# Score products in 64x64 tiles of the array, and the order of a step's work on TensorE, VectorE and ScalarE

## The reference

```
for t in range(S):
    kt, vt, rt = (k[:, :, t], v[:, :, t], r[:, :, t])
    cur = np.einsum('bhd,bhe->bhde', u[None] * kt, vt)
    y[:, :, t] = np.einsum('bhd,bhde->bhe', rt, state + cur)
    state = w[None, :, :, None] * state + np.einsum('bhd,bhe->bhde', kt, vt)
...
x = transposed y, (3072, 384)
logits = x @ phi; d = softmax over tokens; c = softmax over slots
slot_out[e] = relu(slot_input[e] @ w1[e]) @ w2[e];  x = c @ slot_out
h = x @ w_in;  g = h * (1.0 / (1.0 + np.exp(-1.702 * h)));  out = g @ w_out
```

## Time and profile before

| what | value |
|---|---|
| median of three runs | 389.57 us (388.96 to 389.83) |
| profiled execution | 389.61 us, its span 387.8 us, mean granted TensorE clock 0.996 |
| TensorE matmuls busy | 375.5 us, 97% of the span |
| VectorE, ScalarE, GpSimd busy | 229.2, 187.4, 111.7 us |
| moved by DMA | 63.77 MB, of which 58.75 MB read from HBM |
| attention | first 122 us; experts to about 160 us; feed-forward to the end |

### The profile page before, as it was taken

One profiled execution on the slowest core, in us unless ns is written; L12 is line 12 of the kernel. 1 busy time (PEld: TensorE's weight loads), 2 busy tenths in 40 slices (PEclk: granted clock), 3 DMA queues, 4 the chain that ended last, 5 costly groups with the idle time before them and its releaser, 6 DMA issues.

```text
span 387.8 us, 9112 instructions
## 1 busy us (share of the span) xinstructions
PE 375.5 (97%) x3224; PEld 296.0 (76%) x3224; DVE 229.2 (59%) x419; ACT 187.4 (48%) x432; POOL 111.7 (29%) x125
## 2 busy tenths in 40 slices
PE   7889899999999999899999999999999999999996
PEld 6778687877876344578888888888888888888885
DVE  6787778787774301286665565555556655655560
ACT  1235454545444431576655546454655465455552
POOL 5987798887682020144400000000000000000000
PEclk9899999999999999999999999999999999999999
DMA  7999999999999999900002001000200020002002
GB/s 232 289 315 394 382 355 405 403 370 358 402 336 370 328 334 403 378 26 3 0 0 84 0 0 67 16 0 0 81 0 0 0 81 0 0 0 81 0 2 82
DMA packets 28966, 63.77 MB, mean 164 GB/s; under 512 B 3088, under 2 KB 17056, under 8 KB 28560
## 3 DMA queue, kind: packets, MB, share of 16 engines
q1 hardware_dynamic: 27600, 62.99, 44.6%
q10 hardware_dynamic: 1344, 0.49, 0.7%
HBM read 58.75 MB, written 4.72 MB: 164 GB/s over the span
## 4 chain that ended last, share of the span: by engine, by line
PE 79%; DMA 7%; POOL 6%; issue 3%; DVE 2%; SPq 2%; ACT 0%; DVEq 0%; POOLq 0%
PE bank L598 11%; PE bank L597 11%; PE bank L596 11%; PE pair L596 6%; PE pair L598 5%; PE pair L597 5%; PE bank L341 5%; PE pair L380 4%; DMA ring<-win 4%; PE bank L583 4%; DMA krb<-kr 3%; PE pair L371 3%; PE pair L363 3%; PE bank L401 2%; POOL rkn L1046 2%
## 5 line engine op out<-in xcount | busy, mean ns | idle before, releaser
L825 DVE TENSOR_TENSOR gf<-bank,sg 128x512 f32<-128x512 f32 x72 | 49.7, 692 | 63.4 <-ACT sg L993 63.1
L993 ACT ACTIVATE sg<-bank 128x512 f32<-128x512 f32 x72 | 42.9, 598 | 73.3 <-PE bank L583 73.2
L597 PE MATMUL bank<-ghi,whi 128*128 128x512 f32 x192 | 74.7, 389 | 0.0
L596 PE MATMUL bank<-glo,whi 128*128 128x512 f32 x192 | 74.7, 389 | 0.0
L598 PE MATMUL bank<-ghi,wlo 128*128 128x512 f32 x192 | 74.7, 389 | 0.0
L831 DVE TENSOR_TENSOR glo<-gf,ghi 128x512 fp32r<-128x512 f32 x96 | 69.4, 723 | 0.2
L999 ACT ACTIVATE ghi<-gf 128x512 fp32r<-128x512 f32 x96 | 60.0, 625 | 0.9 <-DVE gf L825 0.8
L873 ACT ACTIVATE yt<-pair 112x512 f32<-112x512 f32 x24 | 14.3, 598 | 57.7 <-PE pair L380 57.7
L596 PEld LDWEIGHTS bank<-glo,whi 128*128 128x128 f32 x192 | 36.0, 188 | 7.5
L597 PEld LDWEIGHTS bank<-ghi,whi 128*128 128x128 f32 x192 | 36.0, 188 | 7.5
L598 PEld LDWEIGHTS bank<-ghi,wlo 128*128 128x128 f32 x192 | 36.0, 188 | 7.5
(11 more groups left out here) (162 smaller groups left out, 535.0 us busy)
## 6 DMA issues: line engine op xcount, KB each, us to landing
ring<-w SPq DMA_DIRECT2D x24, 512.0 KB, 6.3
rkb<-rk SPq DMA_DIRECT2D x23, 512.0 KB, 5.4
krb<-kr SPq DMA_DIRECT2D x24, 384.0 KB, 5.6
ring<-w SPq DMA_DIRECT2D x4, 1536.0 KB, 14.5
ring<-w SPq DMA_DIRECT2D x8, 768.0 KB, 10.4
vb<-v SPq DMA_DIRECT2D x24, 192.0 KB, 5.6
out<-ob SPq DMA_DIRECT2D x18, 256.0 KB, 2.1
ring<-win SPq DMA_DIRECT2D x3, 1024.0 KB, 14.1
```

The source lines that it names most:

```text
L596: pe.matmul(o, w_hi, lo, start=(f == 0), stop=False)
L597: pe.matmul(o, w_hi, hi, start=False, stop=False)
L825: dve.tensor_tensor(gf[:, f % 2, :], bank[f % 4][:, :], sg[:, f % 2, :], ALU.mult).then_inc(gf_ok, 1)
L993: act.activation(sg[:, f % 2, :], bank[f % 4][:, :], ACT.Sigmoid, scale=1.702).then_inc(sg_ok, 1)
```

## The change

The scores are cut into halves of their output partitions, 16 products of 48x64 instead of 8 of 48x128. The products of the earlier state with r (`earlier`) leave `outputs` and stand directly ahead of the scores of the next step. The transposes of the bonus values (`bonus_turns`) leave `outputs` too and come last in the step, behind tokens, for the step's own n. So the order becomes earlier(n-1), scores(n), values(n-1), state(n-1), tokens(n-2), bonus_turns(n), and at b = 2 the gathering behind that. Both new groups get waits of their own through an instruction that raises `tiles_go`. VectorE scales step n+1 ahead of the mask of n. ScalarE's decay comes ahead of its columns, and `row_exp` at the end of its step (5,3). GpSimd subtracts the row maximum ahead of the bonus values of (5,3); `vd` is released by a semaphore of its own, `vd_used`.

```diff
@@ scores
+                pe.sem_inc(tiles_go, 1)
                 for hp in range(HP):
-                    for p0, i in HEADS:
-                        s = slice(p0, p0 + D)
-                        last = pe.matmul(SC[i][:, hp * CH:(hp + 1) * CH],
-                                         rks[s, b % 2, 1, hp, :], rks[s, b % 2, 0, hp, :], start=True, stop=True)
+                    for half in HALVES:
+                        for p0, i in HEADS:
+                            s = slice(p0, p0 + D)
+                            last = pe.matmul(SC[i][half, hp * CH:(hp + 1) * CH],
+                                             rks[s, b % 2, 1, hp, half], rks[s, b % 2, 0, hp, :], start=True, stop=True)
...
+            def bonus_turns(c, b):
+                n = B * c + b
                 wait(pe, yt_ok, n)
                 wait(pe, vd_ok, n + 1)
...
+                last.then_inc(vd_used, 1)
+            def earlier(c, b):
+                if is_first(c):
+                    pe.sem_inc(rs_used, 1)
+                else:
+                    wait(pe, s_new, n - 2)
+                    pe.sem_inc(tiles_go, 1)
...
+                    last.then_inc(rs_used, 1)
...
@@ step on TensorE
+                if not is_first(c, b):
+                    earlier(*prev(c, b))
                 scores(c, b)
                 if not is_first(c, b):
+                    if is_first(c):
+                        bonus_turns(*prev(c, b))
                     outputs(*prev(c, b))
...
-                    if tail and b == 2:
-                        gather(c - 1, LG, 2 * c)
                     if not is_first(*prev(c, b)):
                         tokens(*prev(*prev(c, b)))
+                if not is_first(c) or b == B - 1:
+                    bonus_turns(c, b)
+                if tail and b == 2:
+                    gather(c - 1, LG, 2 * c)
...
@@ step on VectorE
+                if is_first(c) and b:
+                    mask(c, b)
+                    scale(*following(c, b))
+                else:
+                    if more:
+                        scale(*following(c, b))
+                    mask(c, b)
+                if more:
+                    bonus_sum(*following(c, b))
...
@@ step on ScalarE
-                if is_last(c) and b == 3:
-                    row_exp(0, EARLY)
                 if not is_first(c, b):
-                    columns(*prev(c, b))
                     if not is_last(prev(c, b)[0]):
                         decay(*prev(c, b))
+                    columns(*prev(c, b))
...
                         rows(*prev(*prev(c, b)))
+                if is_last(c) and b == 3:
+                    row_exp(0, EARLY)
...
@@ step on GpSimd
+                if is_last(c) and b == 3:
+                    pool.wait_ge(rmax_ok, 1)
+                    pool.tensor_tensor(*row_terms(0, 0, EARLY), ALU.subtract).then_inc(csub_ok, 1)
                 bonus_values(c, b)
```

More of the change, by code:

```diff
@@ L38 @@
 HEADS = ((0, 0), (64, 1))
+HALVES = (slice(0, 64), slice(64, P))
 LOWEST = -3.0e38
@@ L184, in rwkv_soft_moe_ffn @@
             sem(n) for n in ("zeroed", "chain", "tables", "wks_done", "wkn_ps", "wkn_ok"))
-        rks_ok, kk_ok, rk_ok, rku_ok, dd_ok, vd_ok, rs_used = (
-            sem(n) for n in ("rks_ok", "kk_ok", "rk_ok", "rku_ok", "dd_ok", "vd_ok", "rs_used"))
+        rks_ok, kk_ok, rk_ok, rku_ok, dd_ok, vd_ok, vd_used, rs_used = (
+            sem(n) for n in ("rks_ok", "kk_ok", "rk_ok", "rku_ok", "dd_ok", "vd_ok", "vd_used", "rs_used"))
         sc_ps, masked, yt_ps, yt_ok, st_ps, sdec, s_new, yn_ps, yn_ok = (
@@ L190, in rwkv_soft_moe_ffn @@
             sem(n) for n in ("lt_ps", "l_ok", "cm_ok", "nm_ok", "ex_ok", "al_ok", "tr_ps", "tr_ok", "p_ps", "run_ok"))
-        nm_new, l_new, mask_go = sem("nm_new"), sem("l_new"), sem("mask_go")
+        nm_new, l_new, mask_go, tiles_go = (sem(n) for n in ("nm_new", "l_new", "mask_go", "tiles_go"))
         spr_ok, bc_ps, nf_ok, fac_ok, lf_ok, ls_ps, samef_ok, rden_ok, si_ps, si_ok = (
@@ L229, in prev, with following @@
             return (c, b - 1) if b else (c - 1, B - 1)
+        def following(c, b):
+            return (c, b + 1) if b < B - 1 else (c + 1, 0)
         def is_first(c, b=0):
@@ L337, in scores @@
                 wait(pe, rks_ok, 2 * n + 2)
+                pe.sem_inc(tiles_go, 1)
                 for hp in range(HP):
-                    for p0, i in HEADS:
-                        s = slice(p0, p0 + D)
-                        last = pe.matmul(SC[i][:, hp * CH:(hp + 1) * CH],
-                                         rks[s, b % 2, 1, hp, :], rks[s, b % 2, 0, hp, :], start=True, stop=True)
-                        if hp == HP - 1:
-                            last.then_inc(sc_ps, 1)
+                    for half in HALVES:
[3 more added lines that the diff above has]
+                                             rks[s, b % 2, 1, hp, half], rks[s, b % 2, 0, hp, :], start=True, stop=True)
+                            if hp == HP - 1 and half == HALVES[1]:
+                                last.then_inc(sc_ps, 1)
                 if is_first(c, b):
@@ L350, in scores @@
                     keep_warm(LG, 4)
-            def outputs(c, b):
+            def bonus_turns(c, b):
                 n = B * c + b
-                if not is_first(c):
-                    wait(pe, s_new, n - 2)
                 wait(pe, yt_ok, n)
@@ L374, in outputs @@
                                                  start=False, stop=False, skip_group_check=True)
-                last.then_inc(rs_used, 1)
+                    last.then_inc(rs_used, 1)
+            def outputs(c, b):
+                n = B * c + b
                 wait(pe, masked, 2 * n + 2)
@@ L465, in spread_weights @@
                 last.then_inc(ct_ps, 1)
+            earlier(C - 1, B - 1)
             outputs(C - 1, B - 1)
@@ L737, in step @@
                 tail = not is_first(c)
[L738 to L750, removed]
+                more = not (is_last(c) and b == B - 1)
                 if tail and b == 1:
                     slot_max(c - 1)
+                if is_first(c) and b:
[7 more added lines that the diff above has]
+                    bonus_sum(*following(c, b))
                 if tail and b == 3:
                     running(c - 1)
-                if not is_first(c, b):
-                    if not is_first(*prev(c, b)) and not is_last(prev(*prev(c, b))[0]):
-                        new_state(*prev(*prev(c, b)))
+                if not is_first(c, b) and not is_last(prev(c, b)[0]):
+                    new_state(*prev(c, b))
                 if is_last(c) and b == 2:
@@ L761, in step @@
                     row_sum(*early)
+            scale(0, 0)
+            dve.tensor_tensor(wks[a, :, :], wk[a, :, :], pw[a, 7, :].unsqueeze(2).to_broadcast([PAIR, HP, CH]),
+                              ALU.mult).then_inc(wks_done, 1)
+            bonus_sum(0, 0)
             steps(dve, step)
-            mask(C - 1, B - 1)
             def low_weights(which, t):
@@ L1059, in bonus_values @@
                 pool.wait_ge(v_in[b], 16 * (c + 1))
-                wait(pool, rs_used, n - 1)
+                wait(pool, vd_used, n - 1)
                 if is_first(c, b):
@@ L1082, in step @@
                         pool.memset(own[:, j, 2, :].bitcast(F32), 0.0).then_inc(own_ok, 1)
-                if is_last(c) and b == 2:
-                    pool.wait_ge(rmax_ok, 1)
-                    pool.tensor_tensor(*row_terms(0, 0, EARLY), ALU.subtract).then_inc(csub_ok, 1)
                 if is_last(c) and b == 3:
```

## The result

The changed kernel takes 391.32 us (median of 8 runs, 389.36 to 392.67) where the kernel before takes 389.36 (8 runs, 388.71 to 389.85): a ratio of 1.0046, 95% interval 1.0027 to 1.0066. It is slower by 0.5%, where 0.9% faster was forecast.

The account below looks back on a forecast made before the run. TensorE was taken to set the pace in attention, DMA 6% behind. Gains of 3.3 + 0.8 + 0.15 - 0.65 = 3.6 us from 389.6 gave 386.0 us; own range 383.8 to 387.8, with rivals 382.6 to 389.2.

Parts of the forecast that it names:

- The step and the chunk: TensorE in attention: a step falls from 4.16 to 3.86 us, a chunk from 18.64 to 17.55 us.
- The rival of tiles two at a time: Scores of each step: half tiles run two at a time, 1.76 us instead of 0.88, kernel about 400 us; chance 0.06.
- The three changes of shape: TensorE's step: tile shape changes three times instead of five, 0.16 us each.
- (c) of the waits: ScalarE's step: decay ahead of columns ends at 1.7 us, columns can start at 2.6, so the order is free.
- The rival that DMA keeps the gain: Attention chunks: DMA holds 391 GB/s, not 403; chunk 18.1 us, kernel 388.2, or 389 with later `krb`; chance 0.22.
- The early part: Chunk from 31 to 51 us and all before it: 0.8 us won, bounds 0 and 2.
- The last chunk: Hidden transposes win 0.15 us; a new wait of about 1.4 us for GpSimd before the weights' transposes loses 0.65.
- The hand-over as a block: From SyncE's restart to `win` landing: 24 us of SyncE and DMA move with the time TensorE reaches the experts.
- The sum: Whole kernel: three chunks, early part, hidden transposes and end wait add to 3.6 us won, giving 386.0 us.
- `tiles_go`: Rival in each step: its two instructions hold back loads, costing what two shape changes saved; 390.2 us; chance 0.08.

Follow-up runs that it names:

- e4: Changed kernel with ScalarE's copy of the outputs (columns) ahead of the decay again in every step; 392.15 us, ratio 1.0041.
- e5: Changed kernel with both order edits, early softmax moved forward at the end and columns ahead of the decay, half scores kept; 391.73 us, ratio 1.0052.
- e9: e6 with 32 added instructions a step on TensorE's queue that only raise a semaphore nobody waits for; 453.48 us.
- e2: Kernel before with its scores alone as 16 products of 48x64, in the old place, with one semaphore instruction ahead; 390.77 us, ratio 1.0022.
- e11: e6 with the values' products cut in two along the tokens, 32 instructions more a step; 391.1 us, ratio 1.0045.
- e1: Changed kernel with its scores as 8 products of 48x128 again, all else as changed; 390.33 us, ratio 1.0005.
- e6: Changed kernel with early softmax moved forward at the end, columns ahead of the decay, and whole 48x128 scores; 388.51 us, ratio 0.9985.
- e12: e6 without the one semaphore instruction a step ahead of the scores; 388.69 us, ratio 0.9999.
- e10: e6 measured again, unchanged; 388.8 us, ratio 0.9990 to the kernel before.
- e8: Changed kernel with half tiles only in steps of even b, whole ones in odd b; 389.91 us, ratio 1.0019.
- e7: Changed kernel with the five pieces of `w1` of chunk 1 asked for behind the last step instead; 392.12 us, ratio 1.0050.
- e3: Changed kernel with the end's early softmax moved forward: ScalarE's exponential first in step (5,3), VectorE's row sum ahead of the running sums; 390.2 us, ratio 1.0024.

## Why the prediction was wrong, point by point

**The step and the chunk: right, one wait missed.** Start to start, earlier products and scores were to take 1.48 us:

```profile
81.67 0.66 PE L383 MATMUL pair<-rks,st 48*48 48x128 f32 x16
...
82.15 1.05 PE L347 MATMUL bank<-rks 48*64 48x128 f32 x32
...
83.13 1.08 PE L395 MATMUL pair<-at,vb 128*48 128x128 f32 x16
...
84.04 0.53 PE L407 MATMUL bank<-vb,kk 128*48 128x48 f32 x16
...
84.50 0.60 PE L416 MATMUL bank<-idt,yt 112*128 112x112 f32 x4
...
84.99 0.65 PE L366 MATMUL pair<-idt,vd 128*112 128x128 f32 x4
```

They take 1.46, and the 32 half tiles run four at a time, 0.98 us. The rival of tiles two at a time, 1.76 us, is out. The rule of the Trainium skill (TensorE: Matmul & The Clock Gate, Part 3, The mechanism), by which the two halves of a head would not overlap, does not agree with this trace. The three changes of shape came as counted.

The chunk was forecast at 17.55 and measured at 17.9, which takes some 1 us from the gain of the three. The missing 0.35 is in the b = 1 step, in (c) of the waits, where I called the decay ahead of the columns free. That holds where ScalarE is idle, not behind the logits:

```profile
55.19 1.00 POOL L1063 TENSOR_TENSOR rkn<-krb 128x384 f32<-128x384 f32 x1
55.23 0.97 DVE L744 TENSOR_TENSOR stat<-stat 128x1 f32<-128x1 f32 x1
...
56.24 0.37 ACT L919 ACTIVATE et<-bank,stat 128x128 f32<-128x128 f32 x1 [2.35 <-DVE stat L744]
...
56.94 1.00 ACT L904 ACTIVATE st<-st,pw 112x48 f32<-112x48 f32 x4
...
57.84 0.58 ACT L895 ACTIVATE yt<-pair 112x512 f32<-112x512 f32 x1
...
58.54 0.41 PEld L366 LDWEIGHTS pair<-idt,vd 128*112 128x112 f32 x4 [0.34 <-issue]
```

VectorE's instruction on one column takes 0.97 us beside GpSimd's, the exponentials come late, the decay behind them, then the columns, and the bonus transposes wait. With the columns first (e4, e5) the chunk is 17.5, what TensorE and DMA were each said to allow. The rival that DMA keeps the gain is out as well: the engines held 402 and 403 GB/s over a chunk.

**The early part: here the prediction failed.** The step reads "the chunk from 31 to 51 us lost 1.3 us to GpSimd, `krb` and one late scale and mask, ... I take 0.8 for it and all before, bounds 0 and 2." It lost 3.9 us instead, so the sign was wrong: 3.0 in the first pass, which the gaps and the lower clock behind them explain (without them it would have won 2), and 0.9 ahead of the loop. The latter stays open; the first logits start between 29.4 and 31.5 us in all kernels here but e9, with no order by the number of instructions. I had counted what the added 32 instructions a step cost the array, and rightly found nothing. I had not asked what they cost the supply. The loop's body is new to TensorE's queue in chunk 1 alone; in chunks 2 to 4 it is there. The DMA queues show instruction loads of 16 KB, from 10 to 60 us five in the changed kernel (first line) and four in the kernel before (second).

```profile
q8 instruction: 5, 0.08, 0.7%
```
```profile
q8 instruction: 4, 0.07, 0.5%
```

The 0.08 MB are small beside 16 MB of data in the same stretch, but they share the engines with them. The traces tell when each of them ran. In the changed kernel, from 32 to 33 and from 40 to 41 us:

```profile
q8 instruction: 1, 0.02, 7.0%
```
```profile
q8 instruction: 1, 0.02, 7.7%
```

By the packets' own times these two ran from 32.36 to 33.48 and from 40.20 to 41.43 us, and TensorE went on at 34.70 and 42.82, 1.22 and 1.40 us after the landings. The gap in the last chunk ended 1.66 us after the landing of a third, at 108.27. So it is everywhere: of the gaps called "issue" between 20 and 135 us in the thirteen profiles other than e9, 25 (0.2 to 2.6 us) end 1.2 to 1.7 us after such a landing, 24 of them in the middle of a group. The nine others (0.2 to 0.7 us) come 4 us or more after one, at the start of a group. And in none of these profiles does such a load run between 50 and 103 us, in the loop's repeats. Other blocks, such as that landed at 48.09, came in time and have no gap behind them. The view doesn't name the engine of that queue; that it is TensorE's follows from these times.

What is shown, then: a gap is TensorE out of instructions until the next block has landed, and more instructions of either kind make such gaps (after, e2, e5, e11 against before, e1, e6, e12, and 0.5 us in e10). What is less sure, from one profile each: half as many make few in the first pass (e8), and with less data in the queue the same instructions lose less (e7). Whether a late block was asked for late or stood behind data is not seen, and the pace of the supply was not measured. The Trainium skill (Runtime: NRT & Kernel Launch, Instruction fetch mechanics) says that each engine's sequencer fetches its instructions by DMA in 16 KiB blocks ahead of use, and that crossing into the next one is mostly hidden. In the kernel before it is; with 32 more instructions a step beside 357 GB/s of data this case does not agree, by 3.2 us.

**The last chunk: right in the wait, blind to the gap.** GpSimd's last product was to end 7.3 us behind the start of step (5,3), at 117.71; TensorE was to wait some 1.4 us.

```profile
123.54 1.26 POOL L1110 TENSOR_TENSOR lnat<-lnat,rm 128x640 f32<-128x640 f32 x1 [3.32 <-DVE rm L738]
...
124.86 0.66 PE L474 MATMUL bank<-idt,lnat 128*128 128x128 f32 x4 [1.14 <-POOL lnat L1110]
```

It ended 7.1 us behind (124.80 against 117.71), the wait was 1.14, and from the start of the step to the transposes were 7.15 us, for 7.4 forecast and 6.76 before: 0.4 lost where 0.65 was booked. The code of the last chunk stands outside the loop and is new again, which gave the gap of 0.80 us at 109.1.

**The hand-over as a block: right.** From SyncE's restart at 137.90 to the landing of `win` at 161.8 are 23.9 us, as before.

```profile
137.90 0.38 SPq L290
...
145.59 16.21 DMA ring<-win
```

**The sum.** Forecast: 3.3 (three chunks) + 0.8 + 0.15 - 0.65 = 3.6 us won. In the profiled execution: 2.4 won in the three chunks, 3.9 lost ahead of them, 1.4 lost behind (the gap of 0.8 and the wait among it): 2.9 lost. Of the rivals I gave for the slower side, half tiles two at a time and `tiles_go`, neither was it.

## What to carry to other kernels

Count instructions as well as passes: an edit that doubles a group's instructions for the same streamed columns can be free in every repetition of a loop and dear in the first, and in code behind the loop, when the DMA engines are full of data. Look for "issue" pieces in the middle of a group, where no semaphore can be the reason, lay the times of the instruction loads beside them, and test with a version that has the same count in another place. When TensorE stands for a couple of microseconds, add the products behind it at half clock to the bill. And take the part that costs out before you judge the rest: both orders with whole tiles came to 388.5 to 388.8 us, 3 us below the same orders with the added instructions, though not clear of the kernel before.

## What the runs showed of the hardware

- An instruction that only raises a semaphore took 0.15 us of TensorE's queue each when 8 or 16 stood in a row (e9), with 0.051 us shown as its duration. Single ones between groups cost nothing measurable (e12).
- TensorE went on 1.2 to 1.7 us after a 16 KB block of instructions had landed, in each of 25 gaps; the transfer of a block took 0.9 to 2.0 us, mostly 1.1.
- Behind a gap of 2.33 us in a busy stretch the granted clock fell to the lower level for some 3 us of products: the gather took 1.51 us instead of 0.85. Gaps of 2.59 (e3), 2.32 (e5) and 2.03 us (e11) were followed by the same; of three of 1.75 to 1.76 us, one was (e3, at 109 us) and two were not (e4 and e5, at 34 us).
- A VectorE instruction on 128x1 elements took 0.97 us instead of 0.16 while a GpSimd product ran over the same time; 0.68 in chunk 1, again beside a GpSimd product. In the four chunks of the loop it began within the time of such a product and ended at most 0.02 us after it. In the kernel before, where it began just ahead of one (88.65 and 88.72 us), it took 0.16.
- The runs of kernels with the added instructions in every step lie 3.3 to 4.8 us apart (e5: 1.7), those of e8 5.2, those of the versions with whole tiles and single values 2.0 to 2.6 (e12: 3.8), those of the kernel before 1.1 in 8 runs and 2.2 to 3.6 in 17 to 32. No kernel is told apart by this.
